# Attention within four plain blocks, a second pass of groups for the first FFN, and nine weight sums made in the groups

## The reference

```
# 1: gated linear attention, batch 4, 8 heads, 768 steps, head size 48
f = sigmoid(f_logit)
state = f[t] * state + outer(k[t], v[t])      # 48 x 48 per head
y[t] = q[t] @ state
x = y as [3072 tokens, 384]
# 2: first FFN, 384 -> 1536 -> 384
x = ((x @ w_a) * (x @ w_b)) @ w_out
# 3: second FFN, 4 experts, 384 -> 1024 -> 384
p = domain_probs / (sum(domain_probs) + 1e-9)
out = sum over e of p[:, e] * (relu(x @ w1[e]) @ w2[e])
```

## Time and profile before

| | us |
|---|---|
| median of three runs (1293.12 to 1294.21) | 1293.82 |
| the profiled execution | 1291.46 |
| its span, first to last instruction | 1289.7 |
| TensorE busy | 1280.1 |
| VectorE busy | 915.8 |
| GpSimd busy | 684.1 |
| ScalarE busy | 635.5 |

### The profile page before, as it was taken

One profiled execution on the slowest core, in us unless ns is written; L12 is line 12 of the kernel. 1 busy time (PEld: TensorE's weight loads), 2 busy tenths in 40 slices (PEclk: granted clock), 3 DMA queues, 4 the chain that ended last, 5 costly groups with the idle time before them and its releaser, 6 DMA issues.

```text
span 1289.7 us, 26428 instructions
## 1 busy us (share of the span) xinstructions
PE 1280.1 (99%) x9319; PEld 1258.5 (98%) x9319; DVE 915.8 (71%) x1775; ACT 635.5 (49%) x1316; POOL 684.1 (53%) x739
## 2 busy tenths in 40 slices
PE   9999999999999999999999999999999999999999
PEld 7999999999999989999999999999999999999998
DVE  8866766767645478767887677787668777677765
ACT  7654444445434455644444554445554455544442
POOL 4336766657656466574444744444744444644440
PEclk9999999999999999999999999999999999999999
DMA  8524445553433143132332242232342332432221
GB/s 258 171 75 147 138 137 153 157 163 117 130 98 128 56 124 93 61 109 87 98 99 81 83 145 83 86 99 61 104 137 85 98 92 66 138 110 87 82 86 38
DMA packets 90324, 140.59 MB, mean 109 GB/s; under 512 B 8848, under 2 KB 64336, under 8 KB 90192
## 3 DMA queue, kind: packets, MB, share of 16 engines
q1 hardware_dynamic: 90192, 138.89, 35.4%
HBM read 119.98 MB, written 22.41 MB: 110 GB/s over the span
## 4 chain that ended last, share of the span: by engine, by line
PE 97%; DVE 1%; DMA 0%; issue 0%; POOL 0%; ACT 0%; SPq 0%; DVEq 0%; ACTq 0%; POOLq 0%
PE bank L2809 10%; PE bank L2810 10%; PE bank L2808 10%; PE bank L2578 10%; PE bank L2580 9%; PE bank L2579 9%; PE bank L2708 6%; PE bank L2706 6%; PE bank L2707 6%; PE score_banks L2708 3%; PE score_banks L2706 3%; PE score_banks L2707 3%; PE bank L2568 2%; PE bank L2572 2%; PE score_banks L2497 1%; PE score_banks L2526 1%
## 5 line engine op out<-in xcount | busy, mean ns | idle before, releaser
L1576 POOL TENSOR_TENSOR wu<-w_r,wu 128x640 fp32r<-128x640 f32 (+1 forms) x156 | 242.4, 1568 | 96.2 <-ACT wu L1084 96.2
L1581 POOL TENSOR_TENSOR wd<-raw,wd 128x384 fp32r<-128x384 f32 x140 | 142.3, 1030 | 272.5 <-ACT wd L1089 272.5
L2120 DVE SCALAR_TENSOR_TENSOR xt<-bank,pn,xt 128x384 f32<-128x384 f32 x288 | 176.8, 615 | 148.7 <-PE bank L2810 143.9
L2808 PE MATMUL bank<-wd,h_hi 128*128 128x384 f32 x768 | 257.6, 335 | 0.0
L2809 PE MATMUL bank<-wd,h_hi 128*128 128x384 f32 x768 | 257.5, 335 | 0.0
L2810 PE MATMUL bank<-wd,h_lo 128*128 128x384 f32 x768 | 257.4, 335 | 0.0
L2708 PE MATMUL bank<-x_lo,wu 128*128 128x384 f32 x479 | 161.5, 337 | 0.0
L2706 PE MATMUL bank<-x_hi,wu 128*128 128x384 f32 x479 | 160.3, 335 | 1.0 <-DVE hb L2025 1.0
L2707 PE MATMUL bank<-x_hi,wu 128*128 128x384 f32 x479 | 160.3, 335 | 0.0
L2578 PE MATMUL bank<-xs_hi,wab 128*128 128x384 f32 x426 | 148.2, 348 | 0.4 <-ACT a_sb L1135 0.4
L2809 PEld LDWEIGHTS bank<-wd,h_hi 128*128 128x128 f32 x768 | 144.2, 188 | 0.0
(11 more groups left out here) (253 smaller groups left out, 2871.5 us busy)
## 6 DMA issues: line engine op xcount, KB each, us to landing
w_r<-weight_sums SPq DMA_DIRECT2D x144, 320.0 KB, 2.9
raw<-w SPq DMA_DIRECT2D x48, 576.0 KB, 4.0
unit<-fkq SPq DMA_DIRECT2D x28, 504.0 KB, 4.6
weight_sums<-w_s SPq DMA_DIRECT2D x18, 384.0 KB, 4.5
v_in<-v_chunks SPq DMA_DIRECT2D x32, 144.0 KB, 4.2
out<-xt SPq DMA_DIRECT2D x24, 192.0 KB, 4.3
weight_sums<-w_s SPq DMA_DIRECT2D x54, 64.0 KB, 4.0
weight_sums<-w SPq DMA_DIRECT2D x40, 64.0 KB, 2.7
```

What stands on the lines that cost most here:

```text
L1576: eng.tensor_tensor(wu_piece(g, n, 1), wu_raw(g, n), wu_piece(g, n, 0).bitcast(f32), ALU.subtract).then_inc(s_ulo, 1)
L1581: eng.tensor_tensor(wd[half(g)][:, 1, n, :], wd_raw(n), wd[half(g)][:, 0, n, :].bitcast(f32), ALU.subtract).then_inc(s_dlo, 1)
L2120: eng.scalar_tensor_tensor(out=acc(b, t), in0=d, scalar=w, in1=acc(b, t), op0=ALU.mult, op1=ALU.add).then_inc(s_acc, 1)
L2808: eng.matmul(o, hh, w_hi, start=(f == fs[0]), stop=False)
```

## The change

`PLAIN` is 4: two FFN1 passes of groups follow, eight groups each, so there are 60 groups in place of 52. Units 4 to 31 are laid into 48 steps in place of 72; the order of every engine but SyncE in the plain part is now written out call by call. Nine of the 18 weight sets stay in the plain part, the others are made by GpSimd in groups 2, 4, 10, 12 and 17 to 21, out of a raw buffer of their own, `raw_s`; to make room, the staging ring of activation sums has five buffers in place of eight. The first exponential of a unit (`exps`) is a call apart from its logarithm. Scores now wait for the states of the unit before. The orders of the groups and hand-overs are new.

```diff
     NB1 = T // TB1
-    PLAIN = 6
+    PLAIN = 4
...
     G = len(GROUPS)
     NS = 2 * NF + NQ
+    NSA = 9
     TT = 2 * TB1 // 128
     PIECE = 2 * DM
...
     VRING = 4
 
-    J = {u: 5 * (u - FIRST) + 8 if u < 2 * PPB else 6 * (u - FIRST) + 5 for u in range(FIRST, NU)}
+    J = {u: 5 * (u - FIRST) + 8 if u < 2 * PPB else 29 + (u - 2 * PPB) * 365 // 100 for u in range(FIRST, NU)}
...
 
+    NEAR = dict(load=-9, v=-4, limit=-6, logs=-5, sums=-5, decays=-4, gates=-3, ends=-3, keys=-2, turn=0, krt=1, scores=2, kv=2, mask=3, state=4, output=6, y=7, store=8)
     FIRST_OF_2 = dict(CLOSE, logs=-7, sums=-6, decays=-5, ends=-4)
 
     SECOND_OF_2 = dict(CLOSE, limit=-9)
     UNIT_AT = {(step, J[u] + after): u for u in J
                for step, after in (FIRST_OF_2 if u == FIRST else SECOND_OF_2 if u == FIRST + 1 else LAST_OF_2 if u == 2 * PPB - 1 else CLOSE if u < 2 * PPB else
-                                   LAST_OF_ALL if u == NU - 1 else TOGETHER).items()}
+                                   NEAR).items()}
     CMIN_AT = J[NU - 1] + 8
     STRONG_AT = CMIN_AT + 9
     PN_AT = 40
...
 
-    SUMS_AT, SUMS_PACE = 31, 9
+    SUMS_G = (2, 4, 10, 12, 17, 18, 19, 20, 21)
+    SUMS_AT, SUMS_PACE, SUMS_LONG = 31, 10, 8
     WU_AT, WD_AT = (3 * FT1 * (PLAIN - 1) + 18, 3 * FT1 * (PLAIN - 1) + 32), 3 * FT1 * (PLAIN - 1) + 29
 
     def x2_at(n):
-        return CMIN_AT + 9 + 2 * n
+        return CMIN_AT + 4 + 1 * n
 
 
...
-        NXT = 8
+        NXT = 5
         x2_t = [None] * NXT
 
+        raw_s = sb(later, "raw_s", [128, KT * FG * 128])
         for n in range(12, NX):
             x_operand(n)
...
 
         def turned(g):
-            p, q = GROUPS[g]
-            after = 2 * NF if PASSES[p][0] == 1 else NQ
-            return q == after - 1 and p + 1 < len(PASSES) or q == NQ and p > 0
+            return any(r[0] < g <= r[-1] for r in ((14, 16), (6, 8), (25, 27), (36, 38), (47, 49)))
 
...
             elif n < 8 or n == 11:
                 attention_done(eng)
+                if n == 3:
+                    eng.wait_ge(s_mint, 1)
             else:
                 eng.wait_ge(s_upb, FT1 * (PLAIN - 1) + max(0, (n - 10) // 2))
...
 
-        def w1_raw(f, k):
-            return raw.rearrange("p a n -> p (a n)")[:, (k * FG + f) * 128:(k * FG + f + 1) * 128]
+        def sum_raw(q):
+            return raw.rearrange("p a n -> p (a n)")[:, 0:KT * FG * 128] if q < NSA else raw_s[:, :]
+
+        def w1_raw(q, f, k):
+            return sum_raw(q)[:, (k * FG + f) * 128:(k * FG + f + 1) * 128]
 
 
...
                     eng.wait_ge(s_ws, 16 * q)
-                dst = raw.rearrange("p a n -> p (a n)")[:, 0:KT * FG * 128].rearrange("p (k f) -> p k f", k=KT)
+                if q == NSA:
+                    eng.wait_ge(s_upb, N1)
+                dst = sum_raw(q).rearrange("p (k f) -> p k f", k=KT)
                 if q < 2 * NF:
...
                 if downs(g) == 0:
-                    eng.wait_ge(s_ws, 16 * NS)
+                    eng.wait_ge(s_ws, 16 * NSA)
                 else:
                     eng.wait_ge(s_dhi, w_downs(g))
...
                     load_w1(0)
                 for q in range(NS):
-                    if j == SUMS_AT + SUMS_PACE * q + 6:
-                        if q + 1 < NS:
+                    if j == SUMS_AT + SUMS_PACE * q + SUMS_LONG and q < NSA:
+                        if q + 1 < NSA:
                             load_w1(q + 1)
                         store_sums(q)
-                    if j == SUMS_AT + SUMS_PACE * q + 4:
+                    if j == SUMS_AT + SUMS_PACE * q // 2 + 4:
                         copy_w1(q)
                 if j == WU_AT[0] - 8:
...
                     load_wd(g + 1)
+                if g + 1 in SUMS_G:
+                    q = NSA + SUMS_G.index(g + 1)
+                    if q > NSA:
+                        store_sums(q - 1)
+                    load_w1(q)
+                elif g == SUMS_G[-1]:
+                    store_sums(NS - 1)
                 if g and GROUPS[g] == (GROUPS[g][0], 0) and ffn(g - 2) == 2:
                     store_out(blocks_of(g - 2))
...
-            def logs(u):
+            def exps(u):
                 t = unit_ring[ring(u)][0:P2, F, :]
                 eng.wait_ge(s_lim, u + 1)
                 eng.activation(t, t, ACT.Exp, scale=-1.0).then_inc(s_exp, 1)
+
+            def logs(u):
+                t = unit_ring[ring(u)][0:P2, F, :]
                 eng.wait_ge(s_exp, u + 1)
                 eng.activation(t, t, ACT.Ln, bias=1.0).then_inc(s_log, 1)
...
                     eng.wait_ge(s_ys, before_in_two(u) + 1)
                 if u >= FIRST:
+                    eng.wait_ge(s_st, states(u, 0))
                     src = unit_ring[ring(u)]
...
 
                 eng.wait_ge(s_krt, min(u + 2, NU))
+                if u == NU - 1:
+                    eng.wait_ge(s_ys, NU - 1)
```

A piece of the new order in the plain part, TensorE's and VectorE's, around units 18 to 20:

```diff
+            up_1(22, 0)
+            output(17)
+            kv(18)
+            scores(18)
+            up_1(22, 1)
+            down_1(21)
+            turn(19)
+            up_1(23, 0)
+            output(18)
+            kv(19)
+            scores(19)
+            up_1(23, 1)
+            down_1(22)
...
+            gate(22)
+            sums(20)
+            h_rest(22)
+            limit(21)
+            mask(19)
+            state(19)
+            gate(23)
+            ends(20)
+            keys(20)
```

TensorE's order in the plain part, the places that the prediction speaks of: `turn(8)` stands after `up_1(8, 0)`, `turn(31)` after `scores(30)` in step 37, `output(31)` between `up_1(39, 0)` and `up_1(39, 1)`. GpSimd's weight sets there: set 7 has two of its operations done before `gates(31)`, the rest and set 8 after it. GpSimd in two of the groups:

```diff
+                elif g == 18:
+                    down_rest(g, 0)
+                    up_rest(g + 1, 0)
+                    up_rest(g + 1, 1)
+                    down_rest(g, 1)
+                    up_rest(g + 1, 2)
+                    for n in range(0, 4):
+                        w_sum(14, n)
+                    down_rest(g, 2)
+                    for n in range(4, 16):
+                        w_sum(14, n)
+                elif g == 19:
+                    down_rest(g, 0)
+                    down_rest(g, 1)
+                    down_rest(g, 2)
+                    up_rest(g + 1, 0)
+                    up_rest(g + 1, 1)
+                    up_rest(g + 1, 2)
+                    for n in range(0, 16):
+                        w_sum(15, n)
```

VectorE in group 1 (in diff form, the operations that move):

```diff
                     add(g, 5)
-                    h1_rest(g, 0)
                     add(g, 6)
                     add(g, 7)
                     add(g, 8)
                     add(g, 9)
                     add(g, 10)
                     product(g, 3)
+                    product(g, 4)
+                    h1_rest(g, 0)
+                    h1_rest(g, 1)
+                    product(g, 5)
+                    h1_rest(g, 2)
+                    h1_rest(g, 3)
+                    h1_rest(g, 4)
+                    h1_rest(g, 5)
+                elif g in (2, 4, 10, 12):
+                    add(g, 1)
```

More of the change, by code:

```diff
@@ new lines, in _ @@
+            h_rest(3)
+            keys(5)
+            mask(4)
+            state(4)
+            gate(4)
+            first_lo(11)
+            first_lo(12)
+            ends(6)
+            h_rest(4)
+            keys(6)
+            first_lo(13)
+            first_lo(14)
+            sums(7)
+            limit(8)
+            limit(9)
+            gate(5)
+            mask(5)
+            state(5)
+            h_rest(5)
+            sums(8)
+            first_lo(15)
+            ends(7)
+            ends(8)
@@ new lines, in _ @@
+            gate(6)
+            keys(7)
+            h_rest(6)
+            mask(6)
+            state(6)
+            first_lo(16)
+            gate(7)
+            keys(8)
+            sums(9)
+            mask(7)
+            state(7)
+            h_rest(7)
+            ends(9)
+            limit(10)
+            keys(9)
+            first_lo(17)
+            gate(8)
+            mask(8)
+            sums(10)
+            h_rest(8)
+            gate(9)
+            limit(11)
+            state(8)
@@ new lines, in _ @@
+            h_rest(9)
+            gate(10)
+            sums(11)
+            ends(10)
+            mask(9)
+            h_rest(10)
+            keys(10)
+            limit(12)
+            state(9)
+            gate(11)
+            ends(11)
+            sums(12)
+            h_rest(11)
+            keys(11)
+            mask(10)
+            limit(13)
+            gate(12)
+            state(10)
+            h_rest(12)
+            ends(12)
+            y_out_1(0)
+            keys(12)
+            sums(13)
@@ new lines, in _ @@
+            gate(13)
+            mask(11)
+            ends(13)
+            state(11)
+            h_rest(13)
+            gate(14)
+            limit(14)
+            keys(13)
+            mask(12)
+            h_rest(14)
+            sums(14)
+            limit(15)
+            gate(15)
+            state(12)
+            h_rest(15)
+            ends(14)
+            probs(2)
+            keys(14)
+            mask(13)
+            state(13)
+            limit(16)
+            gate(16)
+            probs(3)
@@ new lines, in _ @@
+            sums(15)
+            sums(16)
+            h_rest(16)
```

(143 more changed lines are left out.)

1857 lines of the change are left out of this document (1358 added, 499 removed).

## The result

The changed kernel takes 1350.95 us (median of 4 runs, 1345.06 to 1354.37), the kernel before in the same rounds 1293.47: a ratio of 1.044, 95% interval 1.040 to 1.048. I had forecast 1283.1, with 1290 as the upper end. The profiled execution is the shortest of the four, 1345.06 us, and the changed kernel's runs lie 0.7% apart where those of before lie 0.1% apart; so a stage of one trace is good to a few us.

A forecast was written before the change was run, and what follows sets the result against it. TensorE was taken as the bound, busy 1280.1 of 1289.7 us. From 1291.46: -12.8 for fewer matmuls, +1.5 new stalls, +0.5 longer `h_lo` wait, +2.4 from profiled run to median: 1283.1 us, range 1279.5 to 1290.

The forecast's parts named there:

- The count and the pace: TensorE, whole kernel: 72 matmuls fewer, at a steady 173.6 ns each in the groups.
- The saving of 12.8 us: TensorE: 112.8 us of plain steps removed, 100.0 us of groups added, net -12.8 us, all on the path.
- I take 1.5 us of new stalls here: Plain part, attention packed into 48 steps in place of 72: TensorE gains 1.5 us of new stalls.
- the upper bound of 22: Plain part, new stalls: 22 us if VectorE's waits of the kernel before stay; lower bound 0.
- My two rows "without a stall": At 40 to 60 and 617: VectorE busy 18.22 of 20 and 13.60 of 17.2 us, TensorE never standing.
- the price I had given them: Units 8 to 31 in the plain part: 8.78 us of TensorE a unit.
- C: Units 4 to 31: VectorE's mask and `kr` waits prove latency, +21.6 in place of 1.5, 1303.2 us; chance 0.07.
- D's sign: GpSimd late in groups with sums or at hand-over (+5, chance 0.08) would show as `wu` or `x_lo` releasing TensorE.
- Cost 0, bounds 0 and +11: Nine weight sums made by GpSimd in groups: no cost; +11 us if sums run at their slowest mean.
- All at nothing: SP's queue: the sets' added loads and stores, with the next group's `wu` loads behind them, cost nothing.
- The rule that I weighed: GpSimd contends with VectorE for SBUF; mean lengths should fall slightly, 0 to -0.2 us a unit, outside the sum.

The follow-up runs named there:

- the mends: Changed kernel with units' logits loaded ahead, raw weights' loads earlier, and a wait at every sum of sets 13 to 17: 1320.42 us, ratio 1.021.
- the lighter one: Changed kernel with VectorE's limit on 8 and scan on 64 of 384 columns for units 4 and later: 1343.41 us, ratio 1.041.

## Why the prediction was wrong

- **The count and the pace held.** 72 matmuls fewer, and 173.6 ns each where nothing stalls: the rest comes to 752.3 to 753.8 us in every run without starvation, 751.3 by the pace. The saving of 12.8 us is in the count; no run shows it as a shorter time.
- **"I take 1.5 us of new stalls here"** is the step that failed most: the plain part lost 38.9 us, beyond the upper bound of 22. VectorE's share was not the measure. Its work came out as worked out, and the mask waits shrank as said; but I had left out the loads altogether. With units planned 8.8 us apart and four buffers, the load of a unit had to wait for the output product of the unit four before, and then 4.6 us (median) for its data; unit 8's came late for its place in SyncE's list. My two rows "without a stall" could not show this: at 617 there are no units, and at 40 to 60 the buffers were free and the loads early. Shown: loads 10.8 us (the run with logits ahead); VectorE's two shortened operations 6.7 more on top of the mends; GpSimd's sums 4 to 7. Not split further: the 14 us that are left, low clock included; they lie mostly before unit 8's output, and the denser units behind it came to the price I had given them only with work of VectorE and GpSimd taken off.
- **The rivals.** C had the right kind of cause, waits that prove to be latency, and the wrong waits: the two kinds that it counted came to 8.7 us (masks) and 5.2 (`kr`), and the new one was of a kind that the trace of before hardly showed, 1.4 us in two waits of VectorE for loads. Its 21.6 us were over half of what came, in part by luck. D's sign did not come, no `wu` or `x_lo` of GpSimd released TensorE; GpSimd's cost went through VectorE and SyncE.
- **"Cost 0, bounds 0 and +11"** for the sums in groups failed too: without them the time is 24 us less. I asked whether GpSimd has the time (it has: 94.2 us busy of 121 from 579 to 700), not what its operations do to VectorE while they run. That is 13.1 us in the rest: shown, by the seven runs with pauses or short sums, all back at 752 to 754. By traces: no stretched `h_lo` 752.3 to 753.8, one 757.6, two 764.3 to 764.5, three 767.9, four 772.4, so about 5 us each.
- **"All at nothing"** for SyncE's queue: the first sum of a set waited 20.0 us in three sets for a load issued behind the next weights, worth 5.3 us of the groups. Of the groups' other 9, the two added kinds of wait (`hb` and `h_lo`) and one fall of the clock cover most; that isn't separated.
- **The rule that I weighed** (the Trainium skill, "GPSIMD Engine Reference", Key points) was the warning, and I used it only for mean lengths. The Trainium skill has it sharper in "SBUF — State Buffer", section "SBUF: two separate sides": it calls the pair of ports that VectorE and GpSimd share an exclusive lock, which whoever starts first holds for the whole instruction. The traces agree on the kinds of operation hit (two inputs in SBUF, or a copy or an operation with a constant within it), but the wait is not one instruction of 0.49 us: it is 5.7 us, a dozen of them.
- **The clock** was in no term. A stall cost its length and then up to 5 us more.

## What to carry over

Before packing work more densely, follow each buffer's cycle (last reader, issue, landing, first reader) at the new pace, not only each engine's share, and look at the first units apart from the steady ones. Busy shares of 70% don't protect an order of five engines in which each operation waits for another engine; price the round trip. And where GpSimd gets a long row of short operations beside VectorE's critical ones, break the row with a real wait or two: in the second FFN that gave back 11 us, in the plain part nothing.

## What the hardware showed that I had not expected

- Starvation: a VectorE operation of under 1 us took 3.1 to 7.2 us beside a back-to-back row on GpSimd. In the second FFN it was always `h_lo`, and all 14 ended 0.4 us behind the fifteenth sum, where GpSimd waits for its own last operation. It is not certain: of the 30 sets made without added pauses there (six kernels of five), 14 had one, and the kernel before made 17 sets beside the units, in rows up to 13 us long, with none. There some GpSimd operations took 0.6 to 1.1 us in place of 0.46, as if it were GpSimd that gave way. The second FFN agrees: two or three sums took 0.67 to 0.83 us in each of the 16 sets without a starved `h_lo`, one (0.65) in each of the 14 others. What decides who gives way is open. With pauses, 30 sets had none over 2.1 us.
- In the changed kernel TensorE's clock went to 1.2 GHz within or after stalls of 1.85 to 6.2 us, for 3 to 10 us each; others of 2.2 (at 49.99) and 2.7 us (213.44) left it alone.
- The changed kernel's runs scatter by 0.7%, the lighter one's by 2%, the kernel before by 0.1%. That chance starvation is behind it is a guess from the first point.
